# A fused attention and mixture-of-experts kernel: earlier gates, spread first weight loads, a reordered start and last products by row block

## What is computed

```python
# attention: 4 x 8 heads, 576 rows, head size 64
scores = scale * q @ k.T
scores = where(scores >= max(scores) - tau, scores, -1e9)
x = softmax(scores) @ v                  # 2304 tokens x 512
# first mixture: one of 8 experts for each token
logits = normed(x) @ normed(expert_emb).T / moe_tau
e = argmax(logits); gate = softmax(logits)[e]
x = gate * (relu(x @ w1[e]) @ w2[e])     # 512 -> 1024 -> 512
# second block, dense
h = x @ w_in                             # 512 -> 2048
out = (h * tanh(softplus(h))) @ w_out    # 2048 -> 512
```

## Time and profile before

| | |
|---|---|
| time, median of 3 runs | 1135.31 us (1134.59 to 1137.09) |
| the profiled execution | 1136.64 us |
| its span in the trace | 1135.0 us |
| busy: PE, DVE, POOL, ACT | 1050.4, 630.5, 580.4, 509.0 us |
| mean granted TensorE clock | 0.974 of full speed |

### The profile page before, as it was taken

One profiled execution on the slowest core, in us unless ns is written; L12 is line 12 of the kernel. 1 busy time (PEld: TensorE's weight loads), 2 busy tenths in 40 slices (PEclk: granted clock), 3 DMA queues, 4 the chain that ended last, 5 costly groups with the idle time before them and its releaser, 6 DMA issues.

```text
span 1135.0 us, 21549 instructions
## 1 busy us (share of the span) xinstructions
PE 1050.4 (93%) x6536; PEld 872.8 (77%) x6536; DVE 630.5 (56%) x1477; ACT 509.0 (45%) x1035; POOL 580.4 (51%) x680
## 2 busy tenths in 40 slices
PE   6999999999984989789999995799999999999998
PEld 4767777777763877668888884699999999999997
DVE  6787878787844312112222121567767667676664
ACT  4666766666644212112222120345554554545553
POOL 3233333333335477777762331886656556565554
PEclk9999999999995999899999998999999999999999
DMA  4442324322355489988882632620101001010000
GB/s 130 137 137 79 94 71 117 88 77 79 98 172 157 140 271 252 290 277 286 283 287 84 223 120 79 182 73 1 56 1 56 1 0 55 0 55 0 29 1 28
DMA packets 102623, 129.58 MB, mean 114 GB/s; under 512 B 39520, under 2 KB 56928, under 8 KB 102048
## 3 DMA queue, kind: packets, MB, share of 16 engines
q1 hardware_dynamic: 78912, 68.39, 20.2%
q0 software_dynamic: 18880, 53.22, 15.2%
q10 hardware_dynamic: 4768, 7.15, 1.8%
HBM read 112.74 MB, written 15.99 MB: 113 GB/s over the span
## 4 chain that ended last, share of the span: by engine, by line
PE 58%; POOL 6%; DMA 5%; issue 2%; DVE 1%; ACT 1%; POOLq 0%; DVEq 0%; SPq 0%; ACTq 0%
PE ps L1029 17%; PE ps L1031 17%; PE ps L1030 17%; DMA stage<-w 4%; POOL wl L553 3%; PE ps L1055 1%; POOL woutl L553 1%; POOL wh L564 1%; PE ps L969 1%; PE ps L1025 1%; DMA wouth<-w_out 1%; PE ps L1105 1%; PE ps L979 0%; POOL xs_far L590 0%; ACT junk L772 0%
## 5 line engine op out<-in xcount | busy, mean ns | idle before, releaser
L553 POOL TENSOR_TENSOR wl<-stage,wh 128x512 fp32r<-128x512 f32 x128 | 162.0, 1288 | 63.4 <-DMA stage<-w 57.4
L665 POOL TENSOR_TENSOR mg<-mw,mr 128x384 f32<-128x384 f32 x96 | 118.5, 1235 | 74.7 <-DVE mr L1435 74.7
L710 ACT ACTIVATE ex<-sc,rmin 128x576 f32<-128x576 f32 x144 | 111.6, 776 | 95.4 <-DVE sc L1215 94.9
L1029 PE MATMUL ps<-yth,winh 128*128 128x384 f32 x384 | 132.6, 345 | 7.6 <-DVE mw L1423 7.6
L669 POOL TENSOR_TENSOR gl<-mg,gh 128x384 fp32r<-128x384 f32 x96 | 97.6, 1017 | 77.1 <-ACT gh L841 77.1
L1215 DVE TENSOR_SCALAR_CACHE_REDUCE sc<-ps,nscale 128x576 f32<-128x576 f32 x144 | 117.1, 815 | 27.0 <-PE ps L884 22.5
L1031 PE MATMUL ps<-yth,winl 128*128 128x384 f32 x384 | 130.8, 341 | 0.0
L1030 PE MATMUL ps<-ytl,winh 128*128 128x384 f32 x384 | 130.3, 339 | 0.0
L518 POOL TENSOR_SCALAR thr<-rmin,taup 128x1 f32<-128x1 f32 x144 | 67.0, 466 | 104.3 <-DVE sc L1215 103.4
L1031 PE MATMUL ps<-wouth,gl 128*128 128x512 f32 x288 | 114.0, 396 | 0.0
L1030 PE MATMUL ps<-woutl,gh 128*128 128x512 f32 x288 | 113.9, 396 | 0.0
(11 more groups left out here) (201 smaller groups left out, 2366.8 us busy)
## 6 DMA issues: line engine op xcount, KB each, us to landing
wh<-w POOLq DMA_DIRECT2D x32, 1024.0 KB, 9.5
stage<-w SPq DMA_DIRECT2D x128, 256.0 KB, 4.6
y_sorted<-yo ACTq DMA_DIRECT2D x25, 256.0 KB, 3.5
q_t<-qT SPq DMA_DIRECT2D x16, 288.0 KB, 2.9
k_t<-kT SPq DMA_DIRECT2D x16, 288.0 KB, 3.1
vb<-v SPq DMA_DIRECT2D x16, 288.0 KB, 3.4
out<-os SPq DMA_DIRECT2D x18, 256.0 KB, 2.8
stage<-w_in SPq DMA_DIRECT2D x16, 256.0 KB, 3.2
```

Source lines behind the costliest of these rows:

```text
L553: g.tensor_tensor(dst, raw, src.bitcast(F32), ALU.subtract).then_inc(w_split, 1)
L665: g.tensor_tensor(mg[:, f % 2, :], mw[:, f % 2, :], mr[:, f % 2, :], ALU.mult).then_inc(g_done, 1)
L710: act.activation(ex[:, i % 2, t * S:(t + 1) * S], sc[:, i % 2, t * S:(t + 1) * S], ACT.Exp, bias=rmin[:, i % 2, t:t + 1], scale=-1.0).then ...
L1029: pe.matmul(out_, lhs_h, rhs_h, start=start, stop=False)
```

## The change

In the attention stage SP no longer issues the three small loads; ACT does, before its table load, so q_t and k_t come first on SP's queue. The loads of `q_d` have a semaphore of their own, for which only the fifth unit of a step waits. PE makes the scores of unit 0 before the norms of the embeddings. DVE copies the norms out between the first `copy_max` pair and the first `mask`; the rest of the embeddings' operations stand in the last two units of attention. ACT does the first two exponentials before the embeddings' logarithm. POOL issues expert 0's four loads after units 2, 4, 6 and 8. In the expert stage DVE's and ACT's gate operations stand before and directly after slot 0's `low_x`, PE's 18 gate matmuls before `t_h(0)`, and `slot_gates` in slot 0. At the end, `down` of pieces 14 and 15 is split by row block.

```diff
@@ sync
-        sp.dma_start(tauc[:, :], tau).then_inc(tau_in, 16)
-        sp.dma_start(mtau[:, :], moe_tau).then_inc(tau_in, 16)
-        sp.dma_start(emb[:, :, :], embT.rearrange("(k p) e -> p k e", p=P)).then_inc(emb_in, 16)
-            sp.dma_start(q_d[0:DH, par, 0:DH], qT[t, 0, :, PAIRS * P:S]).then_inc(qk_in[par], 16)
-            sp.dma_start(q_d[DH:P, par, DH:P], qT[t, 1, :, 0:DH]).then_inc(qk_in[par], 16)
+            sp.dma_start(q_d[0:DH, par, 0:DH], qT[t, 0, :, PAIRS * P:S]).then_inc(qd_in[par], 16)
+            sp.dma_start(q_d[DH:P, par, DH:P], qT[t, 1, :, 0:DH]).then_inc(qd_in[par], 16)
@@ gpsimd
-                if unit(b, i) == 2:
-                    for q in range(QUARTERS):
-                        load_quarter(0, 0, q)
+                if b == 0 and i in (2, 4, 6, 8):
+                    load_quarter(0, 0, i // 2 - 1)
@@ scalar
+        act.dma_start(tauc[:, :], tau).then_inc(tau_in, 16)
+        act.dma_start(emb[:, :, :], embT.rearrange("(k p) e -> p k e", p=P)).then_inc(emb_in, 16)
+        act.dma_start(mtau[:, :], moe_tau).then_inc(emb_in, 16)
+        exp(0, 0)
         act.wait_ge(norms_e, 2)
...
-        exp(0, 0)
         exp(0, 1)
...
+        act.wait_ge(gate_in, 1)
+        act.activation(lg3[:, :, :], lg2[:, :, :], ACT.Exp).then_inc(gate_exp, 1)
         high_x(0)
         slot(0, True, False)
-        act.wait_ge(gate_in, 1)
-        act.activation(lg3[:, :, :], lg2[:, :, :], ACT.Exp).then_inc(gate_exp, 1)
@@ tensor
             if j == 0:
-                pe.wait_ge(qk_in[st], (body + i // BODY) * 64 + 64)
+                pe.wait_ge(qk_in[st], (body + i // BODY) * 32 + 32)
             wait(pe, max_done, tiles_before(body, i))
             if tiles_of(i) == 1:
+                pe.wait_ge(qd_in[st], (body + i // BODY) * 32 + 32)
...
+        scores(0, 0)
         pe.wait_ge(cvec, 2)
...
-        scores(0, 0)
         scores(0, 1)
...
         t_x(1)
+        pe.wait_ge(gsel_ready, 1)
+        for t in range(NT):
+            m = pe.matmul(ps[:, GS0:GS0 + 3 * SLOTS], sel[:, t, :], ...)
+        m.then_inc(g_mm, 1)
         t_h(0)
...
-        slot(1)
-        pe.wait_ge(gsel_ready, 1)
-        for t in range(NT):
...
-        for i in range(2, SLOTS - 1):
+        for i in range(1, SLOTS - 1):
             slot(i)
...
-        for f in range(NF - LAG, NF):
+        for f in range(NF - LAG, NF - 2):
             down(NG - 1, f, False)
+
+        def down_rows(f, j):
+            pe.wait_ge(gl_ready, (NG - 1) * NF + f + 1)
+            m = passes(ps[:, 2048 + 512 * j:2560 + 512 * j], gh[:, f % 4, j * P:(j + 1) * P],
+                       gl[:, f % 4, j * P:(j + 1) * P], wouth[:, f, :], woutl[:, f, :], False, f == NF - 1)
+            if f == NF - 1:
+                m.then_inc(tail_done, 1)
+
+        for f, j in ((NF - 2, 0), (NF - 2, 1), (NF - 1, 0), (NF - 1, 1), (NF - 2, 2), (NF - 1, 2)):
+            down_rows(f, j)
@@ vector, attention
+                if last and i == BODY - 2:
+                    emb_recip()
+                if last and i == BODY - 1:
+                    emb_scale()
                 norm(b, i)
...
             copy_max(0, i, 0)
             copy_max(0, i, 1)
+            if i == 0:
+                emb_norms()
@@ vector, experts
+        gate_logits()
         low_x(0)
+        gates()
         slot(0, True, False)
-        gates()
-        slot(1, False, False)
-        slot_gates()
-        result(0)
-        with dve.Fori(2, SLOTS - 1) as i:
+        with dve.Fori(1, SLOTS - 1) as i:
             slot(i, False, False)
...
-        dve.wait_ge(down_done, NG * NF)
         for j in range(GT_):
+            dve.wait_ge(tail_done, j + 1)
             rows_out(NG - 1, j)
```

More of the change, by code:

```diff
@@ L258, in build @@
     qk_in = [sem(f"qk_in{i}") for i in range(2)]
+    qd_in = [sem(f"qd_in{i}") for i in range(2)]
     v_in = [sem(f"v_in{i}") for i in range(2)]
@@ L344, in build @@
     os_ready = sem("os_ready")
+    tail_done = sem("tail_done")
     out_stored = [sem(f"out_stored{j}") for j in range(GT_)]
@@ L944, in attention @@
                     transpose(b, i + 2)
+        scores(0, 0)
         pe.wait_ge(cvec, 2)
+        pe.wait_ge(const_gp, 5)
         for k in range(KD):
@@ L1076, in _ @@
         t_x(1)
+        pe.wait_ge(gsel_ready, 1)
+        for t in range(NT):
+            m = pe.matmul(ps[:, GS0:GS0 + 3 * SLOTS], sel[:, t, :], gsel[:, t, :, :].rearrange("p a s -> p (a s)"),
+                          start=t == 0, stop=t == NT - 1)
+        m.then_inc(g_mm, 1)
         t_h(0)
@@ L1083, in slot @@
             t_h(i)
-        slot(1)
-        pe.wait_ge(gsel_ready, 1)
-        for t in range(NT):
-            m = pe.matmul(ps[:, GS0:GS0 + 3 * SLOTS], sel[:, t, :], gsel[:, t, :, :].rearrange("p a s -> p (a s)"),
-                          start=t == 0, stop=t == NT - 1)
-        m.then_inc(g_mm, 1)
-        for i in range(2, SLOTS - 1):
+        for i in range(1, SLOTS - 1):
             slot(i)
@@ L1169, in _ @@
         dve.memset(two[:, :], 2.0).then_inc(const_set, 2)
-        dve.wait_ge(tau_in, 32)
+        dve.wait_ge(tau_in, 16)
         dve.tensor_scalar(nscale[:, :], tauc[:, :], 0.0, -(DH ** -0.5), ALU.is_ge, ALU.mult)
         dve.tensor_scalar(taup[:, :], tauc[:, :], 0.0, None, ALU.max).then_inc(cvec, 1)
-        dve.wait_ge(emb_in, 16)
+        dve.wait_ge(emb_in, 32)
         dve.tensor_tensor(embsq[:, :, :], emb[:, :, :], emb[:, :, :], ALU.mult).then_inc(cvec, 1)
@@ L1193, in norm_recip, with emb_norms, emb_recip, emb_scale @@
             link(dve.reciprocal(out_, r2))
-        dve.wait_ge(norms_e, 1)
-        link(dve.reciprocal(rtau[:, :], mtau[:, :]))
-        dve.tensor_copy(ne[:, :], ps[:, INV0:INV0 + E]).then_inc(norms_e, 1)
+        def emb_norms():
+            dve.wait_ge(norms_e, 1)
+            dve.tensor_copy(ne[:, :], ps[:, INV0:INV0 + E]).then_inc(norms_e, 1)
+        def emb_recip():
+            dve.wait_ge(rec_e, 1)
+            norm_recip(ne[:, :], er0[:, :], er1[:, :], er2[:, :], er0[:, :])
+            link(dve.reciprocal(rtau[:, :], mtau[:, :]))
+        def emb_scale():
+            link(dve.tensor_scalar(er2[:, :], er0[:, :], rtau[:, :], None, ALU.mult))
+            dve.tensor_tensor(embn[:, :, :], emb[:, :, :], er2[:, :].unsqueeze(1).to_broadcast([P, KD, E]),
+                              ALU.mult).then_inc(emb_scaled, 1)
         dve.wait_ge(const_gp, 7)
@@ L1201, in _ @@
         dve.tensor_copy(lane_b[:, :], lane_f[:, :])
-        dve.wait_ge(norms_e, 2)
-        dve.wait_ge(rec_e, 1)
-        norm_recip(ne[:, :], er0[:, :], er1[:, :], er2[:, :], er0[:, :])
-        link(dve.tensor_scalar(er2[:, :], er0[:, :], rtau[:, :], None, ALU.mult))
-        dve.tensor_tensor(embn[:, :, :], emb[:, :, :], er2[:, :].unsqueeze(1).to_broadcast([P, KD, E]),
-                          ALU.mult).then_inc(emb_scaled, 1)
         def copy_max(body, i, t):
@@ L1337, in _, with gate_logits @@
         dve.tensor_copy(pos_i[:, :], posf[:, :])
-        def gates():
+        def gate_logits():
             dve.wait_ge(gate_ln, 2)
@@ L1344, in gates @@
                               ALU.mult).then_inc(gate_in, 1)
+        def gates():
             dve.wait_ge(gate_exp, 1)
@@ L1383, in slot @@
                 low_x(i + 1)
-            if not first and not (isinstance(i, int) and i == 1):
+            if first:
+                slot_gates()
+            else:
                 result(i - 1)
```

## The result

The changed kernel takes 1117.54 us (median of four runs, 1116.24 to 1119.63), beside 1134.95 for the kernel before (four runs, 1133.91 to 1137.09): a ratio of 0.9846 with an interval of 0.9825 to 0.9867, 17.4 us less. The forecast was 17.7 less.

A forecast was written before the change was run, and what follows sets the result against it. POOL's chain was taken to bound the kernel up to 492.61 us, PE's own work afterwards. Gains of 12.0 + 2.7 + 1.9 + 1.1 = 17.7 took 1135.31 to 1117.6 us, range 1113.6 to 1122.0.

The forecast's parts named there:

- the bounding argument: Expert stage up to 492.61: POOL's chain sets the time, with PE stalling 17.95 us for its low parts; afterwards PE does.
- Part 1: Expert stage: early gates remove POOL's wait for gslot, sixteenth gather 11.98 us earlier; worth 12.0, bounds 8 to 13.
- forecast milestone: Expert stage: gsel near 364.8, gates_kept near 371.8, fifteenth gather ending at 374.42, sixteenth starting at 374.72.
- part 2: Start: q_t and k_t issued first, PE's first scores some 2.8 us earlier; worth 2.7, bounds 2.0 to 3.6.
- part 3: Attention's first units: spreading expert 0's loads removes DVE's idle hole at unit 3; worth 1.9, bounds 0.9 and 2.1.
- upper bound: Start: worth 3.6 us if PE, busy from 4.8 without a gap, leaves its slow matmuls one unit earlier.
- rival A: POOL's chain: stretched stage loads or a wait on PE give back 4 to 8 us; 1121.6 to 1125.6; chance 0.14.
- the other end: Expert stage: faster stage DMAs, with fewer bytes left behind them, add 1 us to the gates' worth, so 13.
- rival C: From 480 on: lower granted PE clock; slower than before beyond 2.8% loss, 1143 us at 4%; chance 0.03.
- Part 4: Kernel's end: two copies, 1.2 us, leave the path, against 0.1 to 0.2 of stall; worth 1.1, bounds 0.8 and 1.2.
- rival E: Attention's first units: each of four load issues waits for a 0.82 us DVE operation; 1120.7 us; chance 0.07.

The follow-up runs named there:

- part 2 alone: Kernel before with only the new start: small loads on ACT's queue, q_d's own semaphore, scores first, embeddings' operations late; span 1131.7 us.
- part 3 alone: Kernel before with only expert 0's four loads spread after units 2, 4, 6, 8; spans 1139.3 and 1134.4 us; a third execution issued them ahead of row_sums.
- the kernel with the gates alone: Kernel before with only the early gate operations, gate product and slot_gates; start, first loads and end as before; 1126.26 us, ratio 0.9932.
- The fastest kernel: Changed kernel with the five last gathers (slots 20 to 24) issued after the loop over experts instead of after expert 2; 1110.49 us, ratio 0.9796.

## Why the prediction was right, and where it was not

The total was right within 0.3 us of the measured difference (17.7 against 17.4), and the bounding argument held: until slot 9 the kernel's time is POOL's. That it came so close is partly luck: parts 2 and 3 were put 1.7 us too high, and 2.5 us that no term of the sum held came on POOL's way to slot 9. That is the account of one pair of executions; the others behind the median of 17.4 (15.1 to 19.9 by the interval of the ratio) have no traces. By the pair:

**Part 1 (12.0).** The sixteenth gather gained 14.48, of which 2.92 were there at the first gather: 11.56 for the gates. Every forecast milestone held: `gsel` was made ahead of slot 1, the gates came at 369.11, 2.80 us before the fifteenth gather ended, where 2.6 of room was forecast. Two of the three stalls stayed, at 3.92 and 1.55 where "about 2 to 4 and 5" was forecast. The second was shorter because the chain gained more on its way. The experiment with the vector work alone shows that moving that work was not enough, and that the product's place on PE, with the operations behind it, had to move too.

**Parts 2 and 3 (4.6 together).** This is the term that was mis-sized: 2.92 us had come of it at the first gather. Of the forecast's 4.6, 3.77 were there at the last norm of attention, and 0.85 went between that norm and the first gather (30.14 us before, 30.99 after), where the prediction had put nothing. The means over the executions, with their number in brackets, are:

| | first scores | last norm | first gather |
|---|---|---|---|
| neither part (6) | 6.94 | 323.99 | 354.40 |
| part 2 alone (1) | 5.20 | 322.11 | 352.76 |
| part 3 alone, issues ahead of or behind `row_sums` (3) | 6.85 | 321.47 | 351.73 |
| both (3; the one with late small loads left out) | 5.45 | 320.90 | 351.54 |

At the first gather part 3 alone has 2.7 us and both parts together 2.9, so part 2 adds 0.2 to part 3 there, though alone it had 1.6. Part 3 gave its 2.05 exactly where it was put; the part that fell short is part 2. Of the forecast 2.8 at the first scores 2.05 came in this pair, and 1.5 in the mean. Two reasons. The first keys took 4.1 us to land (1.36 to 5.5), where the 3.1 of the earlier trace rows was taken, a median over two loads of which none was the first thing on its queue. And the old start had a wait that the prediction named and did not price as chance: `q_d`, which released the first scores at anything from 6.45 to 7.61. The forecast started from the latest of these.

From the first scores to unit 3, the new start gives back 0.4 in the mean, but not where the 0.2 to 0.4 for the norms had been allowed. From the copy of unit 0 to that of unit 1, where the norms stand, it takes 4.05 to 4.06 us against 3.94, and loses 0.1. From the copy of unit 1 to that of unit 2 it takes 3.80 to 4.21 (mean 4.07) against 3.48 to 4.20 (mean 3.74) in the nine executions with the old start. That stretch goes with the eight matmuls of unit 2's scores, which take 1.76 to 2.17 us with the new start and 1.24 to 2.15 with the old one. Timeline of PE, the changed kernel and then the kernel with only the vector work early:

```profile
13.92 2.07 PE L886 MATMUL ps<-k_t,q_t 64*128 64x288 f32 x8
```

```profile
14.62 1.24 PE L884 MATMUL ps<-k_t,q_t 64*128 64x288 f32 x8
```

As its upper bound the prediction allowed that PE, busy earlier, leaves its slow matmuls one unit earlier. It did not: these eight still took most of their slow time in all four kernels with the new start, and in four of the nine old ones they had none. That is also about half of why the two parts do not add: the three executions of part 3 alone took 3.48 to 3.61 us for this stretch, and the three with both parts 4.11 to 4.21.

**What came on top.** POOL's pieces for slot 9 gained 2.5 us more than the gather did. In the stretch of expert 4's loads, POOL waits 2.84 us in one wait and 3.11 in another ahead of it for the stage DMAs, and the timeline of the kernel before has four such waits there:

```profile
464.64 5.28 POOL L553 TENSOR_TENSOR wl<-stage,wh 128x512 fp32r<-128x512 f32 x4 [3.59 <-DMA stage<-w]
...
475.65 1.30 POOL L553 TENSOR_TENSOR wl<-stage,wh 128x512 fp32r<-128x512 f32 x1 [0.56 <-DMA stage<-w]
480.50 1.28 POOL L553 TENSOR_TENSOR wl<-stage,wh 128x512 fp32r<-128x512 f32 x1 [3.55 <-DMA stage<-w]
482.22 3.79 POOL L553 TENSOR_TENSOR wl<-stage,wh 128x512 fp32r<-128x512 f32 x3 [0.44 <-DMA stage<-w]
```

They sum to 8.14 us, against 5.95. The prediction feared longer waits here (rival A), and allowed 1 us of gain as the other end. Why they shrank is not shown. That fewer bytes compete with the stage loads once the gathers are done earlier would be a reason, but the kernel with the gates alone speaks against it: its sixteenth gather is 11.7 us earlier than before, and after its sixteenth POOL waits for stage DMAs for 23.9 us in all, against 23.5 in the kernel before and 20.8 in the changed one. From the sixteenth gather to PE's restart at slot 9 it takes 106.95 us, the kernel before 105.91, the changed one 103.41, and the nine executions with late gates and the gathers in their old place lie between 103.89 and 106.44. So 2.5 us is also what this stretch varies by among kernels in which nothing of it was changed, and chance may be all of it.

**The clock, twice, with opposite signs.** After the short pause of 1.55 us at 475.63 PE went on at full clock (1.00 from 476 to 488), where after the 4.94 us of the earlier trace rows it had 0.89 (493 to 505): slot 9's result is 18.30 us earlier where its start was 16.98. The last slot gave that back. Busy time by stage, the changed kernel from 673 to 680 and the kernel before from 691 to 698:

```profile
673.00:680.00 7.00, 6.92 (x23) 5.50 (x24) 0.00 (x0) 0.00 (x0) 0.00 (x0) 0.76 0.00 0
```

```profile
691.00:698.00 7.00, 5.78 (x24) 4.43 (x24) 0.86 (x2) 0.00 (x0) 0.00 (x0) 1.00 0.03 9
```

Both kernels pause for 1.79 us before the last slot's second product, and only the changed one then ran a part of it at the lower of the clock's two levels: 10.07 us from the last but one result to the last in place of 8.44. The fastest kernel has 1.00 there, with the same code. With so few executions it can't be called the change's cost; rival C, a clock lower for good, did not happen (0.99 from 479 to 677).

**Part 4 (1.1).** From the last matmul to the end 5.14 became 3.81, a gain of 1.33; the stall for the last `gl` is 0.14 (the matmul at 1111.56 comes 0.36 after its neighbour, not 0.22 to 0.23). Net 1.2. Another 0.85 between the last slot's result and the last matmul (16.66 to 15.67, less the stall) was lost in places that were not followed.

The whole, in us: 2.92 + 11.56 + 2.50 + 1.32 - 1.64 - 0.64 - 0.35 + 1.33 = 17.0, where 0.64 lies between the last result and the first pieces of `w_out` and 0.35 between these and the last matmul.

**The price of rival E.** The rival took the stretch of POOL's threshold beside a mask (0.28 to 0.74) for what an issue would suffer. The Trainium skill ("SBUF — State Buffer", "SBUF: two separate sides", the trap in which DVE blocks a GpSimd DMA) says that GpSimd can't write the descriptors of its DMAs while DVE runs an operation in a two-port performance mode. By the section "Who interferes with whom" of the same page that leaves out this kernel's copies, a form of `tensor_scalar` that also writes out its accumulator, and its masks, whose two SBUF inputs contend only with a GpSimd instruction that reads SBUF. The trace agrees: four issues cost POOL 0.79 to 0.96 us each, beside masks and beside copies alike, and no run here shows such an issue waiting for a DVE operation of this kernel's form. The row that the prediction set against the rival, the piece at 82.12 in the earlier trace rows, pointed the right way, but it is a weaker row than it seemed: the piece lies beside two copies (81.72 and 82.66) and ends before the next mask (83.86).

## What to carry to other kernels

When an in-order engine's chain sets the time, follow it back to the one wait that isn't for something it released itself, and see which engines' orders stand behind that wait: here three had to be reordered together, and with two of them alone POOL still waited 15.92 us. Then look for work in the chain that nobody needs yet: moving five gathers out of it was worth another 6 to 7 us by the medians and ratios, in one line. The first wait here, whose end is decided by DMA landings, varied by 1.2 us between executions, so size what is won at a kernel's start from several of them. The same holds inside the chain: 2.5 us of the gain in the traces are no more than one stretch varies by.

## What the runs showed that was not expected

- The first 288 KB load of keys lands 3.8 to 4.2 us after its issue at 1.36, the small loads issued beside it on ScalarE's queue 3.4 to 4.2 after theirs. In the kernel before, the same small loads, first on SyncE's queue and ahead of the large ones, took 2.0 to 2.3. Taking two of them away again made the keys earlier by 0.1 to 0.4 us only, so the small loads suffer from the large ones more than the other way round.
- The time of the first scores varies with the same code from 6.45 to 7.61 us.
- Waits of 0.8 to 5.3 us on ScalarE or DVE, marked "remote", come between 366 and 376 us in eight of the fourteen profiled executions, in the kernel before as in edited ones, while POOL issues gathers; the eight are those that stand alone. Some are hidden, some cost 5 us. What they wait for is open.
- After pauses of PE of 0.5 and 1.55 us the granted clock was 1.00 in the 12 us that followed; after 3.92, 4.94 and 9.65 us it was 0.77, 0.89 and 0.84; after a pause of 1.79 us it was 0.76 in one execution and 1.00 in two others.
